# Second layer's routing logits in three column groups of TensorE, transposed once, with shorter rounds of work

## The chip, the cores and the metric

## The reference, cut to what matters

Banded attention (4 batches, 8 heads, 768 positions, 64 numbers a head) gives x, 3072 tokens of 512 numbers. Then a first layer of experts, each of which takes exactly 384 tokens in the order of all logits, and a second layer with free routing. The second layer's logits are what the change touches:

```python
def _moe2_ref(x, w_skip, w_gate, w1, w2):
    skip_score = x @ w_skip
    do_compute = skip_score > 0
    out = x.copy()
    xc = x[do_compute]
    logits = xc @ w_gate
    e_idx = np.argmax(logits, axis=1)
    ...
    for e in range(E):
        mask = e_idx == e
        h = np.maximum(xc[mask] @ w1[e], 0.0)
        y[mask] = gate_w[mask, None] * (h @ w2[e])
    out[do_compute] = xc + y
```

x there is the first layer's output. There are 8 experts (E), 512 features (DM, KC = 4 chunks of 128) and 1024 hidden numbers (F, FC = 8 chunks).

## The kernel before, in words

The program is one block with a hand-written stream of instructions for each engine; semaphores tie them. There is no scheduler: each engine does its instructions in the order in which they stand.

After the attention come eight **searches**, one for each expert of the first layer in the order in which they fill (`search` on VectorE, `window` on TensorE, from 166 to 573 us). A search finds the logit at which an expert has 384 tokens, in ROUNDS = 17 rounds. In a round VectorE counts how many logits reach each of three candidates (`junk`, L913), TensorE adds the counts over the partitions (L1370), and VectorE makes the next candidates. Then follow a total (L1380), the ranks of the chosen tokens (L1384, L1385), and the list of their ids (L1321, L1329). The next search starts with a transpose of the masked logits (L1364). `window` writes this down for TensorE, and between these steps it calls `work(units)`.

`work` takes items from the list WORK, in order, as long as their units fit into what `room` has allowed so far. WORK holds the first layer's products: 32 items "first" for an expert (L1297, 3 units each), 24 items "second" (L1311, 4 units), "rows" (L1286, the transposes of the gathered rows, 2 units each) and the items "tail", in which the second layer's logits are made. An expert has three tiles (CT = 3) of 128 tokens. The tail of expert k-1 stands among the first 16 items of expert k (`expert_items`): transposes of the output tiles `yb` into the PSUM tiles `XB`, copied by ScalarE to `yT` (`y_features`, L703), then the products of `yT` with the gate weights `wg2` into the PSUM tile `LP`, which ScalarE copies to L2 (L738). `wg2` has 9 real columns (8 experts and the skip weight), padded to 128 with zeros. The work lags behind the searches, so the tails of the first six experts are done in the searches three to eight, the seventh's after them, in `work(sum(...))`, and the eighth's at the end, between the halves of layer one of the second layer's first tile (L1421). Behind the seventh's tail stands the item "totals" (L1397), for which VectorE must have counted the tokens of the first 18 tiles; VectorE in turn waits (`tok_c`) for GpSimd's `keep_ids`, and that for the scatter of the seventh expert's outputs (L564).

The second layer takes tiles of 128 tokens, each with the weights of one expert: `layer1` (L1421, two halves), ScalarE's copies to `h2T` (L752), `x2_transpose` (L1410) and `layer2` (L1432).

Of the kernel before, what the change touches and what calls it, by code (L numbers as in the profile page):

```python
# [5 lines left out]
def banded_attention_two_moe_layers(nc, qT, kT, vwin, vblk, g1, w1a, w2a, skip2, g2, w1b, w2b, out):  # L6
    fp32, bf16, i32 = mybir.dt.float32, mybir.dt.bfloat16, mybir.dt.int32
    ALU = mybir.AluOpType
    ACT = mybir.ActivationFunctionType
# [6 lines left out]
    DM, E = g1.shape  # L16
# [19 lines left out]
    KC = DM // 128  # L36
    FC = F // 128
    CT = CAP // 128
# [6 lines left out]
    WIDE = 128  # L45
# [8 lines left out]
    ROUNDS = 17  # L54
# [5 lines left out]
    with ctx:  # L60
        def sb(name, shape, dt=fp32):
            return ctx.enter_context(nc.sbuf_tensor(name, shape, dt))
# [22 lines left out]
        wg1 = sb("wg1", [128, KC, WIDE + E * (TB - 1)])  # L85
        wg2 = sb("wg2", [128, KC, WIDE])

# [51 lines left out]
        def sba(name, shape, dt=fp32):  # L139
# [27 lines left out]
        yb = sb("yb", [128, CT, DM])  # L167
        yT = sb("yT", [128, 2, KC, 128])

# [58 lines left out]
            onehot_ready blk_ready id_mm idp_ready ids_ready tok_c  # L228
            xg_in xg_tr xgT_ready w_in0 w_in1 w2_in0 w2_in1 h_mm h_act y_mm y_evac y_tr yT_ready l2_mm l2_evac y_out y_st y_written
            gate_sub gate_exp rows8_ready base8_mm teA_ready onehot2_ready id2_mm gid2_ready route2_ready  # L230
# [408 lines left out]
        def _(act):  # L639
# [59 lines left out]
            def y_features(ph, j):  # L699
                act.wait_ge(s["y_tr"], CT * ph + j + 1)  # L700
                if j == 2:
                    act.wait_ge(s["l2_mm"], CT * ph + 1)
                a.activation(yT[:, j % 2, :, :], XB[(j + 1) % 2][:, :].rearrange("p (c t) -> p c t", c=KC),  # L703
                             ACT.Copy).then_inc(s["yT_ready"], 1)
# [10 lines left out]
            def expert(ph, last):  # L715
# [19 lines left out]
                if not last:  # L735
                    hidden(ph + 1, 1)
                act.wait_ge(s["l2_mm"], CT * (ph + 1))
                a.activation(L2[:, bass.ds(CT * ph, CT), :],  # L738
                             LP[:, 0:CT * (E + 1)].rearrange("p (j e) -> p j e", j=CT), ACT.Copy).then_inc(s["l2_evac"], 1)

# [423 lines left out]
        def _(pe):  # L1164
# [84 lines left out]
            def expert_items(k):  # L1249

                head = [("first", k, i, 3) for i in range(16)]
                if k > 0:
                    head[8:8] = [("tail", k - 1, 3, 4), ("tail", k - 1, 4, 4)]
                    head[4:4] = [("tail", k - 1, 1, 4), ("tail", k - 1, 2, 2)]
                    head[0:0] = [("tail", k - 1, 0, 4)]
# [15 lines left out]
            def room(w):  # L1271

                if w == 1:
                    return [0] + [0, 0, 6] + [6] * (ROUNDS - 3) + [15, 28, 4, 8]
                return [8] + [9] * ROUNDS + [15, 28, 4, 6 if w < 5 else 8]

# [158 lines left out]
            def tail(part, tp):  # L1435
# [13 lines left out]

                def y_logits(j):  # L1450
                    if j == 0:
                        pe.wait_ge(s["l2_evac"], START + tp)
                    pe.wait_ge(s["yT_ready"], START + CT * tp + j + 1)
                    for c in range(KC):
                        ins = mm(LP[:, (E + 1) * j:(E + 1) * j + WIDE], yT[:, j % 2, c, :], wg2[:, c, :],  # L1455
                                 start=(c == 0), stop=(c == KC - 1))
                    ins.then_inc(s["l2_mm"], 1)

                if part == 0:
                    y_transpose(0)  # L1460
                    y_transpose(1)
                elif part == 1:
                    y_logits(0)
                elif part == 2:
                    y_transpose(2)
                elif part == 3:
                    y_logits(1)
                elif part == 4:
                    y_logits(2)

# [6 lines left out]
            layer1(0, 0, 1, 0)  # L1477
            for part in range(1, 5):
                tail(part, E - 1)
            layer1(0, 0, 1, 1)  # L1480

            for b in range(KA):
# [60 lines left out]
```

## Time and profile before

| | us |
|---|---|
| median of 3 runs | 910.58 |
| lowest, highest | 905.64, 912.84 |
| the profiled execution, its time | 909.39 |
| its span, first to last instruction | 907.6 |
| TensorE busy in it | 860.7 |
| VectorE busy | 467.2 |
| ScalarE busy | 210.4 |
| GpSimd busy | 219.9 |

All profile times are from the one profiled execution, counted from the start of its span. "PE" is TensorE's matmuls, "PEld" its loads of stationary tiles. In a timeline a row is a run of like instructions: start, length until the last of them ends, engine, line, operation, tiles, stationary and moving shapes, count, and in brackets the idle time before it with what ended it. A window's row has, after its length, each engine's busy time with the number of its instructions, the granted clock of TensorE (1.00 is 2.4 GHz, 0.50 is 1.2 GHz), the DMA engines' share and GB/s.

### The profile page before, as it was taken

Reading aid. Unit: us, or ns where it says so; the run is one execution under the profiler, and the core shown is the slowest. Engines: PE = TensorE matmul, PEld = TensorE weight load, DVE = VectorE, ACT = ScalarE, POOL = GpSimd, SP = SyncE. Lnnn points to the kernel's source line nnn. Section 1 sums busy time; section 2 is a strip of 40 time slices with the busy share of each in tenths; the row PEclk is TensorE's granted clock in tenths of the full one; section 3 lists DMA queues with packets and bytes.
Section 4 is the critical chain, followed back from the end, with each engine's and each line's share of the span. In section 5 each row is a group of like instructions: output and inputs, shape, how many; then the busy total and the mean of one; then the engine's idle time right before and its main releaser. Section 6 shows DMA issues by size and latency. Waiting matters only on the chain.

```text
span 907.6 us, 15611 instructions
## 1 busy us (share of the span) xinstructions
PE 860.7 (95%) x5204; PEld 587.5 (65%) x5204; DVE 467.2 (51%) x2118; ACT 210.4 (23%) x662; POOL 219.9 (24%) x321
## 2 busy tenths in 40 slices
PE   4899999798899999999999999999999999999997
PEld 4789888686346455464646555564877776867775
DVE  8688886577777676667677676160270000000000
ACT  4456665320102121211202121221110111101010
POOL 3578875001030120203021020302012121212111
PEclk8799999899999999999999999999999999999999
DMA  7987751345070522507061431646788989888880
GB/s 206 273 234 213 228 162 48 116 164 188 33 257 34 198 92 89 189 12 266 24 239 51 163 126 56 220 178 208 238 291 324 344 311 337 304 333 321 316 299 15
DMA packets 69271, 174.78 MB, mean 193 GB/s; under 512 B 6064, under 2 KB 10672, under 8 KB 69216
## 3 DMA queue, kind: packets, MB, share of 16 engines
q1 hardware_dynamic: 54600, 143.99, 46.3%
q0 software_dynamic: 6960, 21.69, 6.9%
q10 hardware_dynamic: 7656, 8.36, 2.8%
q8 instruction: 35, 0.57, 0.3%
q14 instruction: 20, 0.16, 0.1%
HBM read 149.19 MB, written 23.59 MB: 190 GB/s over the span
## 4 chain that ended last, share of the span: by engine, by line
PE 78%; DVE 12%; DMA 5%; issue 3%; POOL 2%; ACT 1%; SPq 0%; DVEq 0%; POOLq 0%; ACTq 0%
PE bank L1297 15%; PE bank L1311 15%; PE bank L1421 14%; PE bank L1432 14%; DVE junk L913 3%; PE bank L1182 3%; PE bank L1204 3%; PE bank L1191 2%; PE bank L1455 2%; DMA vw<-vs 2%; PE bank L1218 2%; PE bank L1370 1%; DMA kc<-in_kT 1%; PE bank L1447 1%; PE bank L1286 1%
## 5 line engine op out<-in xcount | busy, mean ns | idle before, releaser
L1297 PE MATMUL bank<-xgT,W 128*128 128x384 f32 x512 | 179.9, 496 | 0.6 <-ACT xgT L686 0.6
L1311 PE MATMUL bank<-W,hT 128*128 128x512 f32 x384 | 178.8, 602 | 0.0
L913 DVE TENSOR_SCALAR_CACHE_REDUCE junk<-Vt,cand 128x192 bf16<-128x192 f32 x376 | 136.1, 410 | 4.8
L1421 PEld LDWEIGHTS bank<-x2T,W 128*128 128x128 f32 x1152 | 131.4, 192 | 7.7 <-issue 7.7
L1421 PE MATMUL bank<-x2T,W 128*128 128x128 f32 x1152 | 131.8, 275 | 0.0
L1432 PE MATMUL bank<-W,h2T 128*128 128x512 f32 x288 | 126.6, 592 | 0.0
L1297 PEld LDWEIGHTS bank<-xgT,W 128*128 128x128 f32 x512 | 90.3, 190 | 53.4 <-issue 3.6
L1070 DVE SCALAR_TENSOR_TENSOR o<-bank,gate,x 128x512 f32<-128x512 f32 x18 | 13.4, 750 | 211.6 <-PE bank L1432 211.6
L1311 PEld LDWEIGHTS bank<-W,hT 128*128 128x128 f32 x384 | 67.1, 190 | 58.0 <-issue 56.0
L1432 PEld LDWEIGHTS bank<-W,h2T 128*128 128x128 f32 x288 | 53.3, 190 | 60.3 <-issue 60.3
L651 ACT ACTIVATE pr<-bank,nmx 128x120 f32<-128x120 f32 x192 | 66.7, 364 | 34.2 <-DVE nmx L819 19.2
L752 ACT ACTIVATE h2T<-bank 128x512 f32<-128x512 f32 x36 | 21.5, 597 | 220.0 <-PE bank L1421 220.0
L691 ACT ACTIVATE hT<-bank 128x384 f32<-128x384 f32 x64 | 31.4, 490 | 150.3 <-PE bank L1297 150.3
L1182 PEld LDWEIGHTS bank<-kw,qz 128*128 128x128 f32 x384 | 55.8, 209 | 1.7
L471 POOL TENSOR_TENSOR pr<-pr,rinv 128x480 f32<-128x480 f32 x48 | 47.3, 985 | 33.4 <-DVE rinv L825 32.0
L1182 PE MATMUL bank<-kw,qz 128*128 128x120 f32 x384 | 55.2, 291 | 0.0
L280 POOL TENSOR_TENSOR hot_id<-hot,pnum 128x384 bf16<-128x384 f32 x7 | 8.2, 1166 | 186.7 <-DVE hot L977 186.7
L928 DVE TENSOR_SCALAR_CACHE_REDUCE reached<-bank 128x7 f32<-128x7 f32 x120 | 19.9, 166 | 62.1 <-PE bank L1370 60.2
L595 POOL COPY now_s<-sidx 128x1 int32 (+1 forms) x18 | 3.3, 183 | 193.3 <-DVE o L1070 193.3
L1370 PEld LDWEIGHTS bank<-cnt,same_e 128*128 128x128 bf16 x136 | 13.2, 97 | 50.7 <-DVE junk L913 45.1
L557 POOL DMA_INDIRECT xg<-x_rows,gidx x24 | 23.6, 985 | 91.3 <-DVE gidx L893 86.4
L564 POOL DMA_INDIRECT out<-yb,tok_i x24 | 23.6, 985 | 84.1 <-ACT yb L695 81.3
(262 smaller groups left out, 1076.8 us busy)
## 6 DMA issues: line engine op xcount, KB each, us to landing
W<-in_moe_w SPq DMA_DIRECT2D x52, 2048.0 KB, 8.0
vw<-in_vwin SPq DMA_DIRECT2D x16, 576.0 KB
qc<-in_qT SPq DMA_DIRECT2D x16, 384.0 KB, 6.6
kc<-in_kT SPq DMA_DIRECT2D x16, 384.0 KB, 7.8
vb<-in_vblk SPq DMA_DIRECT2D x16, 384.0 KB, 6.8
x_rows<-xr SPq DMA_DIRECT2D x24, 256.0 KB, 2.1
y_rows<-yb ACTq DMA_DIRECT2D x24, 256.0 KB
vw<-vs ACTq DMA_DIRECT2D x14, 144.0 KB
```

The lines of the kernel that those rows point to most:

```text
L471: g.tensor_tensor(pr[:, n % NP, :, :], pr[:, n % NP, :, :], rinv[:, n % NP, :].unsqueeze(2).to_broadcast([128, GW, KW]), ALU.mult) \
L557: g.indirect_dma_start(out=xg[:, j, :], out_offset=None, in_=x_rows, in_offset=bass.IndirectOffsetOnAxis(ap=gidx[:, j:j + 1], axis=0)) \
L564: g.indirect_dma_start(out=out, out_offset=bass.IndirectOffsetOnAxis(ap=tok_i[:, j:j + 1], axis=0), in_=yb[:, j, :], in_offset=None).then_ ...
L651: ins = a.activation(pr[:, n % NP, w, :], SC[n % 3][:, KW * w:KW * w + KW], ACT.Exp, scale=SCALE, bias=nmx[:, n % NP, w:w + 1], accum_out= ...
L691: a.activation(hT[:, r, :], HB[r % 2][:, 0:CAP], ACT.Relu).then_inc(s["h_act"], 1)
L913: ins = ve.tensor_scalar(junk[:, c, :], Vt[:, :], cand[:, c:c + 1].bitcast(fp32), 0.0, ALU.is_ge, ALU.add, accum_out=cnt[:, c:c + 1])
L1182: ins = mm(SC[n % 3][:, KW * w:KW * w + KW], qz[u % 2][:, GW * gr + w, :], kw[u % 2][:, GW * gr + w, :], start=False, stop=(w == GW - 1))
L1204: ins = mm(OB[n % 2][D * j:D * j + D, QW * w:QW * w + QW], vw[i][:, GW * gr + w, D * j:D * j + D], pT[:, n % 2, 128 * w + QW * j:128 * w + ...
L1297: ins = mm(HB[r % 2][:, 0:CAP], w1[:, c, 128 * r:128 * r + 128], xgT[:, c, :], start=(c == 0), stop=(c == KC - 1))
L1311: ins = mm(YB[j % 2][:, :], hT[:, r, 128 * j:128 * j + 128], w2[:, r, :], start=(r == 0), stop=(r == FC - 1))
L1421: ins = mm(HB2[h][:, 128 * c:128 * c + 128], W1[:, par, k * F + at:k * F + at + 128], x2T[par][:, k, :], start=(k == 0), stop=(k == KC - 1))
L1432: ins = mm(YB2[par][:, :], h2T[:, f, :], W2[:, par, f * DM:f * DM + DM], start=(f == 0), stop=(f == FC - 1))
```

## The change

The gate weights become the stationary operand, in 32 columns instead of 128, and `yT` the moving one. The three tiles of an expert write to partitions 0 to 31, 32 to 63 and 64 to 95 of `LP`, chunk by chunk in turn. ScalarE copies the 96x128 result to `l2T`, TensorE transposes it back, and ScalarE copies the real columns to L2. `yT` has three buffers instead of two. The tail has four parts instead of five: part 0 the transposes of two tiles, part 1 that of the third, part 2 all logits, part 3 the transpose of the result. They weigh 4, 2, 4 and 1 units instead of 4, 4, 2, 4 and 4, and stand before the first-layer items 0, 4, 8 and 10. The rounds' units alternate between 9 and 8 for fourteen rounds instead of always 9; the last entry of a search is 8 units but for the third search (4), where it was 6 for the third to fifth.

```diff
@@ -83,7 +83,8 @@
         iotaS = sb("iotaS", [128, NSLOT])
         cnt128 = sb("cnt128", [128, NT])
         wg1 = sb("wg1", [128, KC, WIDE + E * (TB - 1)])
-        wg2 = sb("wg2", [128, KC, WIDE])
+        wg2 = sb("wg2", [128, KC, 32])
+        l2T = sb("l2T", [CT * 32, 128])
 
 
         LM = sb("LM", [128, NT, E])
@@ -165,7 +166,7 @@
         xgT = sb("xgT", [128, KC, CAP])
         hT = sb("hT", [128, FC, CAP])
         yb = sb("yb", [128, CT, DM])
-        yT = sb("yT", [128, 2, KC, 128])
+        yT = sb("yT", [128, CT, KC, 128])
 
 
         R2 = sb("R2", [128, NT, NV, NSLOT], bf16)
@@ -226,7 +227,7 @@
             recip_ready norm_done sum_eps gaps_ready prob_tr prob_evac pv_done o_evac xr_tr xr_evac x_st0 x_st1 x_st2 x_st3
             logit_mm logit_in v_ready v_tr cnt_ready cnt_mm tau_diag tau_mm expert_ready expert_read rows_ready base_mm slot_ready
             onehot_ready blk_ready id_mm idp_ready ids_ready tok_c
-            xg_in xg_tr xgT_ready w_in0 w_in1 w2_in0 w2_in1 h_mm h_act y_mm y_evac y_tr yT_ready l2_mm l2_evac y_out y_st y_written
+            xg_in xg_tr xgT_ready w_in0 w_in1 w2_in0 w2_in1 h_mm h_act y_mm y_evac y_tr yT_ready l2_mm l2T_ready l2_tr l2_evac y_out y_st y_written
             gate_sub gate_exp rows8_ready base8_mm teA_ready onehot2_ready id2_mm gid2_ready route2_ready
             gidx_now sidx_now x2_in0 x2_in1 x2_in2 x2_in3 x2_tr x2T_ready te_ready h2_mm h2_act
             y2_mm o2_ready o2_out0 o2_out1 vec pool_c passed""".split()
@@ -698,9 +699,7 @@
 
             def y_features(ph, j):
                 act.wait_ge(s["y_tr"], CT * ph + j + 1)
-                if j == 2:
-                    act.wait_ge(s["l2_mm"], CT * ph + 1)
-                a.activation(yT[:, j % 2, :, :], XB[(j + 1) % 2][:, :].rearrange("p (c t) -> p c t", c=KC),
+                a.activation(yT[:, j, :, :], XB[(j + 1) % 2][:, :].rearrange("p (c t) -> p c t", c=KC),
                              ACT.Copy).then_inc(s["yT_ready"], 1)
 
             def gate_exp(first, count, n):
@@ -734,9 +733,12 @@
                 y_features(ph, 2)
                 if not last:
                     hidden(ph + 1, 1)
-                act.wait_ge(s["l2_mm"], CT * (ph + 1))
+                act.wait_ge(s["l2_mm"], ph + 1)
+                a.activation(l2T[:, :], LP[0:CT * 32, 0:128], ACT.Copy).then_inc(s["l2T_ready"], 1)
+                act.wait_ge(s["l2_tr"], ph + 1)
                 a.activation(L2[:, bass.ds(CT * ph, CT), :],
-                             LP[:, 0:CT * (E + 1)].rearrange("p (j e) -> p j e", j=CT), ACT.Copy).then_inc(s["l2_evac"], 1)
+                             LP[:, 128:128 + CT * 32].rearrange("p (j e) -> p j e", j=CT)[:, :, 0:E + 1],
+                             ACT.Copy).then_inc(s["l2_evac"], 1)
 
             x_features(0)
             hidden(0, 0)
@@ -1250,8 +1252,9 @@
 
                 head = [("first", k, i, 3) for i in range(16)]
                 if k > 0:
-                    head[8:8] = [("tail", k - 1, 3, 4), ("tail", k - 1, 4, 4)]
-                    head[4:4] = [("tail", k - 1, 1, 4), ("tail", k - 1, 2, 2)]
+                    head[10:10] = [("tail", k - 1, 3, 1)]
+                    head[8:8] = [("tail", k - 1, 2, 4)]
+                    head[4:4] = [("tail", k - 1, 1, 2)]
                     head[0:0] = [("tail", k - 1, 0, 4)]
                 items = head + [("first", k, i, 3) for i in range(16, HID)] + [("second", k, i, 4) for i in range(CT * FC)]
                 if k + 1 < E:
@@ -1272,7 +1275,7 @@
 
                 if w == 1:
                     return [0] + [0, 0, 6] + [6] * (ROUNDS - 3) + [15, 28, 4, 8]
-                return [8] + [9] * ROUNDS + [15, 28, 4, 6 if w < 5 else 8]
+                return [8] + [9, 8] * 7 + [9] * 3 + [15, 28, 4, 4 if w == 2 else 8]
 
             def load_x(k, j):
                 if j == 0:
@@ -1447,26 +1450,21 @@
                         ins = tr(XB[(j + 1) % 2][:, 128 * c:128 * c + 128], yb[:, j, 128 * c:128 * c + 128], ident[:, :])
                     ins.then_inc(s["y_tr"], 1)
 
-                def y_logits(j):
-                    if j == 0:
-                        pe.wait_ge(s["l2_evac"], START + tp)
-                    pe.wait_ge(s["yT_ready"], START + CT * tp + j + 1)
-                    for c in range(KC):
-                        ins = mm(LP[:, (E + 1) * j:(E + 1) * j + WIDE], yT[:, j % 2, c, :], wg2[:, c, :],
-                                 start=(c == 0), stop=(c == KC - 1))
-                    ins.then_inc(s["l2_mm"], 1)
-
                 if part == 0:
                     y_transpose(0)
                     y_transpose(1)
                 elif part == 1:
-                    y_logits(0)
+                    y_transpose(2)
                 elif part == 2:
-                    y_transpose(2)
+                    pe.wait_ge(s["l2_evac"], START + tp)
+                    pe.wait_ge(s["yT_ready"], START + CT * (tp + 1))
+                    for c in range(KC):
+                        for j in range(CT):
+                            ins = mm(LP[32 * j:32 * j + 32, 0:128], wg2[:, c, :], yT[:, j, c, :], start=(c == 0), stop=(c == KC - 1))
+                    ins.then_inc(s["l2_mm"], 1)
                 elif part == 3:
-                    y_logits(1)
-                elif part == 4:
-                    y_logits(2)
+                    pe.wait_ge(s["l2T_ready"], tp + 1)
+                    tr(LP[:, 128:128 + CT * 32], l2T[:, :], ident[0:CT * 32, 0:CT * 32]).then_inc(s["l2_tr"], 1)
 
             pe.wait_ge(s["const_ready"], 1)
             pe.wait_ge(s["const_in"], 32)
@@ -1475,9 +1473,10 @@
             work(sum(u for _, _, _, u in WORK))
             tail(0, E - 1)
             layer1(0, 0, 1, 0)
-            for part in range(1, 5):
-                tail(part, E - 1)
+            tail(1, E - 1)
+            tail(2, E - 1)
             layer1(0, 0, 1, 1)
+            tail(3, E - 1)
 
             for b in range(KA):
                 if b >= 1:
```

TensorE, rounds of the seventh search, before the change; `yb` is an output tile to be transposed, `wg,yT` the logits, `xgT,W` first-layer products:

```order
L1455 MATMUL bank<-wg,yT 128x128 x4
L1447 MATMUL bank<-ident,yb 128x128 x4
L1370 MATMUL bank<-cnt,same_e 128x128
L1297 MATMUL bank<-xgT,W 128x384 x3
L1370 MATMUL bank<-cnt,same_e 128x128
L1297 MATMUL bank<-xgT,W 128x384
L1455 MATMUL bank<-wg,yT 128x128 x8
L1370 MATMUL bank<-cnt,same_e 128x128
L1297 MATMUL bank<-xgT,W 128x384 x3
```

and with the change, where lines 1447, 1455, 1370, 1297 are 1450, 1463, 1373, 1300 and the logits' transpose is 1467:

```order
L1450 MATMUL bank<-ident,yb 128x128 x4
L1300 MATMUL bank<-xgT,W 128x384
L1373 MATMUL bank<-cnt,same_e 128x128
L1300 MATMUL bank<-xgT,W 128x384 x3
L1373 MATMUL bank<-cnt,same_e 128x128
L1463 MATMUL bank<-yT,wg 32x128 x12
L1300 MATMUL bank<-xgT,W 128x384
L1373 MATMUL bank<-cnt,same_e 128x128
L1300 MATMUL bank<-xgT,W 128x384
L1467 MATMUL bank<-ident,l2T 128x96
L1300 MATMUL bank<-xgT,W 128x384 x2
L1373 MATMUL bank<-cnt,same_e 128x128
```

The twelve calls of the logits are now in one round with one product, and the transpose is in the next.

TensorE, the seventh expert's tail and the first total (`row,tri`), before:

```order
L1447 MATMUL bank<-ident,yb 128x128 x8
L1297 MATMUL bank<-xgT,W 128x384 x4
L1455 MATMUL bank<-wg,yT 128x128 x4
L1447 MATMUL bank<-ident,yb 128x128 x4
L1297 MATMUL bank<-xgT,W 128x384 x4
L1455 MATMUL bank<-wg,yT 128x128 x8
L1397 MATMUL bank<-row,tri 128x8
L1398 MATMUL bank<-row,ones_bf 128x8
L1297 MATMUL bank<-xgT,W 128x384 x24
```

and with the change:

```order
L1450 MATMUL bank<-ident,yb 128x128 x8
L1300 MATMUL bank<-xgT,W 128x384 x4
L1450 MATMUL bank<-ident,yb 128x128 x4
L1300 MATMUL bank<-xgT,W 128x384 x4
L1463 MATMUL bank<-yT,wg 32x128 x12
L1400 MATMUL bank<-row,tri 128x8
L1401 MATMUL bank<-row,ones_bf 128x8
L1300 MATMUL bank<-xgT,W 128x384 x2
L1467 MATMUL bank<-ident,l2T 128x96
L1300 MATMUL bank<-xgT,W 128x384 x22
```

The first total now has all logits before it and their transpose, with two products, behind it.

TensorE, the eighth expert's tail among the second layer's first tile (`x2T,W`), before:

```order
L1447 MATMUL bank<-ident,yb 128x128 x8
L1421 MATMUL bank<-x2T,W 128x128 x16
L1455 MATMUL bank<-wg,yT 128x128 x4
L1447 MATMUL bank<-ident,yb 128x128 x4
L1455 MATMUL bank<-wg,yT 128x128 x8
L1421 MATMUL bank<-x2T,W 128x128 x16
L1410 MATMUL bank<-ident,x_1 128x128 x4
L1432 MATMUL bank<-W,h2T 128x512 x8
```

and with the change:

```order
L1450 MATMUL bank<-ident,yb 128x128 x8
L1424 MATMUL bank<-x2T,W 128x128 x16
L1450 MATMUL bank<-ident,yb 128x128 x4
L1463 MATMUL bank<-yT,wg 32x128 x12
L1424 MATMUL bank<-x2T,W 128x128 x16
L1467 MATMUL bank<-ident,l2T 128x96
L1413 MATMUL bank<-ident,x_1 128x128 x4
L1435 MATMUL bank<-W,h2T 128x512 x8
```

The logits now follow the third tile's transposes at once, and their own transpose stands behind the second half of layer one.

ScalarE at the same place, before:

```order
L697 DMA y_rows<-yb 128x512
L703 ACTIVATE yT<-bank 128x512 x3
L738 ACTIVATE L<-bank 128x27
L752 ACTIVATE h2T<-bank 128x512 x2
L712 ACTIVATE x2T<-bank 128x512
L708 ACTIVATE t<-t 128x48
```

and with the change:

```order
L698 DMA y_rows<-yb 128x512
L702 ACTIVATE yT<-bank 128x512 x3
L737 ACTIVATE l2T<-bank 96x128
L739 ACTIVATE L<-bank 128x27
L754 ACTIVATE h2T<-bank 128x512 x2
L711 ACTIVATE x2T<-bank 128x512
L707 ACTIVATE t<-t 128x48
```

The copy to `l2T` is added; it and the copy to L stand ahead of the first copy to `h2T`.

## Rows read from the trace of the kernel before

**Rows 1.** The page: the chain that ended last, by engine.
```profile
PE 78%; DVE 12%; DMA 5%; issue 3%; POOL 2%; ACT 1%; SPq 0%; DVEq 0%; POOLq 0%; ACTq 0%
```

**Rows 2.** TensorE in windows: the third, the fourth and the seventh search.
```profile
263.45:315.52 52.07, 51.11 (x216) 1.00 0.35 126
315.52:367.18 51.66, 50.70 (x215) 1.00 0.36 125
470.33:521.91 51.58, 51.20 (x216) 1.00 0.36 130
```

**Rows 3.** TensorE's timeline, rounds of the seventh search.
```profile
478.61 0.22 PE L1370 MATMUL bank<-cnt,same_e 128*128 128x128 bf16 x1
...
480.42 0.23 PE L1370 MATMUL bank<-cnt,same_e 128*128 128x128 bf16 x1 [0.29 <-DVE junk L913]
...
493.01 0.22 PE L1370 MATMUL bank<-cnt,same_e 128*128 128x128 bf16 x1
...
493.77 1.95 PE L1455 MATMUL bank<-wg,yT 128*128 128x128 f32 x16
495.55 0.22 PE L1370 MATMUL bank<-cnt,same_e 128*128 128x128 bf16 x1
...
497.60 0.22 PE L1370 MATMUL bank<-cnt,same_e 128*128 128x128 bf16 x1
```

**Rows 4.** TensorE's timeline, a group of the attention.
```profile
80.69 0.69 PE L1204 MATMUL bank<-pT,vw 120*64 120x64 f32 x16 [0.25 <-DMA vw<-vs]
```

**Rows 5.** TensorE's timeline, around the rank matmuls of that search.
```profile
512.69 5.31 PE L1311 MATMUL bank<-W,hT 128*128 128x512 f32 x12
517.93 0.77 PE L1321 MATMUL bank<-hot_blk,hot_id 128*32 128x24 bf16 x24
518.62 1.13 PE L1311 MATMUL bank<-W,hT 128*128 128x512 f32 x2
```

**Rows 6.** The chain of waits: start, length, what.
```profile
589.18 4.51 DMA out<-yb,tok_i
...
614.13 5.15 PE bank L1311 x12
```

**Rows 7.** TensorE's timeline, the seventh expert's last routing logits.
```profile
594.94 1.95 PE L1455 MATMUL bank<-wg,yT 128*128 128x128 f32 x16
598.34 0.18 PE L1397 MATMUL bank<-row,tri 128*128 128x8 bf16 x1 [1.45 <-DVE row L1081]
```

**Rows 8.** TensorE's timeline, the last expert's routing logits.
```profile
640.88 0.60 PE L1447 MATMUL bank<-ident,yb 128*128 128x128 f32 x4
641.32 2.01 PE L1455 MATMUL bank<-wg,yT 128*128 128x128 f32 x16
...
647.17 7.03 PE L1432 MATMUL bank<-W,h2T 128*128 128x512 f32 x16
```

**Rows 9.** ScalarE's timeline, the same place.
```profile
641.52 0.60 ACT L703 ACTIVATE yT<-bank 128x512 f32<-128x512 f32 x1 [3.68 <-PE bank L1447]
...
643.45 0.59 ACT L752 ACTIVATE h2T<-bank 128x512 f32<-128x512 f32 x1
```

**Rows 10.** TensorE's timeline, four of its waits.
```profile
15.58 0.36 PE L1179 MATMUL bank<-band,spread 67*128 67x480 bf16 x1 [2.17 <-DVE kw L800]
...
34.08 1.12 PE L1204 MATMUL bank<-pT,vw 120*64 120x64 f32 x16 [2.35 <-issue]
...
166.14 0.30 PE L1364 MATMUL bank<-ident,V 128*128 128x128 f32 x1 [3.03 <-DVE V L900]
...
216.94 0.23 PE L1370 MATMUL bank<-cnt,same_e 128*128 128x128 bf16 x1 [1.48 <-DVE junk L913]
```

**Rows 11.** Windows: all engines; PEclk is TensorE's granted clock.
```profile
16.60:26.70 10.10, 7.17 (x43) 6.24 (x42) 7.63 (x20) 4.71 (x25) 6.28 (x8) 0.50 0.55 161
33.70:40.40 6.70, 6.32 (x50) 5.78 (x51) 4.49 (x11) 3.01 (x15) 5.67 (x8) 0.50 1.04 276
166.80:173.50 6.70, 5.48 (x27) 5.42 (x28) 3.98 (x25) 2.14 (x4) 0.00 (x0) 0.50 0.21 78
```

## The prediction

> **What bounds the kernel now.** I read the chain that ended last first: TensorE holds 78% of it, VectorE 12% [rows 1]. So a TensorE microsecond is worth one wherever TensorE is not waiting, and the question is where it would wait. The windows tell that. From the third search on, a search with an expert's products woven in takes 51.6 to 52.1 us, of which TensorE is busy 50.7 to 51.2, at full granted clock [rows 2]. The timeline of the seventh search shows what sets a round. A round begins with the count matmul (L1370); VectorE then tests three candidates, while TensorE works off the round's units. Where TensorE has little to do it waits for VectorE's `junk`: the round from 478.61 to 480.42 is 1.81 us, with 0.29 us of visible wait. That is the floor of a round. A round of three first-layer products takes 2.05 us (495.55 to 497.60); the round with one such product and eight logit calls (16 records) takes 2.54 (493.01 to 495.55) [rows 3]. Hence a first-layer product costs about 0.65 us and the count matmul about 0.11. A second-layer product is 0.86 (12 records in 5.15) [rows 6].
>
> There are eight places with routing logits, one for each expert. Six of them (experts one to six) lie in the rounds of searches three to eight; the seventh and the eighth come after the searches, and they behave differently.
>
> **What the change removes and adds, for one expert.** Removed: 12 calls that load a 128x128 stationary tile and move 128 columns, 24 records. 16 of them take 1.78 us from 493.77 to 495.55 [rows 3], so 0.111 each and 2.67 for 24. Added: 12 calls with 32 stationary columns and 128 moving ones, writing to three partition groups, then a transpose of one record.
>
> The trace has no call with 32 stationary float columns. The nearest is the attention's product with the values, 64 stationary and 64 moving columns, in two partition groups in turn. Its 16 records are busy for 0.69 us, the last of them for about 0.22, so they start within 0.47, 0.03 apart [rows 4]. In a single row 64 columns would take half of 0.111, 0.056. So two streams do run side by side, with float data. They read about as much in a unit of time as three streams with 32 weight columns would: there 256 numbers of a partition (2 x 64 weights, 2 x 64 moving) in 0.06 us, here 480 (3 x 32 and 3 x 128) in 0.111. I take three streams side by side: 8 steps of 0.111 make 0.89. Bounds: nothing side by side, 24 x 0.111 = 2.67; all records at the attention's spacing, 24 x 0.03 = 0.72.
>
> Going over to narrow stationary tiles has a price. The rank matmuls (L1321, 32 columns wide) start 5.24 us after 12 second-layer records that elsewhere take 5.15 [rows 5, 6], so 0.09 to go over; I take 0.09 again for the way back. The logits then cost 1.07 (0.90 to 2.85). The added transpose is one record, 0.11 (four take 0.44) [rows 8]. **Saved: 2.67 - 1.18 = 1.49 us an expert.** Eight times that, 11.9, is the most the change can give.
>
> At TensorEngine Tiling (Array Packing), section Key Properties, the Trainium skill says that a change of tiling mode drains TensorE; the 0.09 in [rows 5, 6] agrees. The Trainium skill's page TensorE: Matmul & The Clock Gate, section Measured speedup vs the span model, gives 2.38 times for three column tiles, not 3. By that the eight steps would be 1.12 instead of 0.89, and the sum below some 1.6 us less gain.
>
> **In the rounds of searches three to eight.** By the order of instructions a whole search holds the same set of products before and after, so TensorE's work falls by 1.49, but its waits at the floor grow. Before, the seventh search has one short round (four row transposes and one second-layer product: 0.44 + 0.86 + 0.11 = 1.41 against 1.81, 0.40 of waiting). After, it has that one and a second, with only two first-layer products: 0.11 + 1.30 = 1.41, another 0.40. The round with the new logits and one product is 0.11 + 1.07 + 0.65 = 1.83, just on the floor: a faster stream gives nothing there, a slower one costs one for one. Net 1.49 - 0.40 = 1.1 for each of searches five to eight, 4.3 together. The cuts of searches three and four fall on other items. The third saves 1.49 and gives a second-layer product (0.86) to the fourth, but two of its rounds fall partly under the floor and its end comes before VectorE's next masked logits: an estimated 0.6 to 0.7 of waiting, net 1.7. The fourth saves 1.49, takes that product, and loses the wait of about 0.4 with which it ends now: 1.1. **Sum 7.1 us.** The sections after the rounds stay as they are from the fifth search on.
>
> What hides the new steps: ScalarE must copy 96x128 numbers between logits and transpose. Two first-layer products and a count matmul stand between, 1.4 us; the copy starts some 0.25 after the last matmul and takes under 0.6, as ScalarE's copy of 512 columns does [rows 9]. I cost it at nothing; uncovered it would be 0.8 for each expert. The three `yT` buffers remove one wait of ScalarE and add none. SyncE's and GpSimd's queues get nothing new. VectorE's smaller fill of `wg2` at the start lies before a wait for the first keys: nothing.
>
> **The seventh expert.** Here TensorE waits already: after the last logits 1.45 us, until 598.34, for VectorE's `row` [rows 7]. The chain behind goes over the scatter of expert seven's last output tile (a DMA of 4.51 us) [rows 6], then `tok_i` on GpSimd and VectorE's counting. None of it is shortened. TensorE arrives 1.6 us earlier (1.49, and the transpose now stands two products behind the wait) and waits 1.6 longer: 3.05 us. Gain zero, and the transpose behind it is a loss of 0.11.
>
> **The eighth expert.** Now one set of logits follows its transposes at once, all three tiles needed: `yT` is ready 0.64 after the transposes start plus 0.60 [rows 8, 9], so TensorE stands about 0.7. It had stood 0 there. Logits 1.07, 32 records, the transpose. Then a new tie: ScalarE is in order, and its copy of the first half of `h2T`, now at 643.45 [rows 9], stands behind the copy of the logits, that is behind the transpose after the second half of layer one. The half ends near 641.3 + 1.07 + 3.57 (32 records of 0.111) = 645.9; with the transpose, the copies and their delays ScalarE frees `h2T` at about 646.9, and the second-layer products start near 646.95 instead of 647.17 [rows 8]. Gain 0.2 of a possible 1.49. VectorE gets the last logits some 2.9 us later, at 646.4. The second total wants its counting only behind the first tile's second-layer products, which last 7.03 us from 647.17 [rows 8]; the same counting, GpSimd's copies with it, took 4.7 us from the end of the DMA (593.7) to 598.34 [rows 6, 7]. It fits.
>
> Sum: 7.1 - 0.1 + 0.2 = **7.2 us off**, if the clock holds.
>
> **The granted clock.** The wait grown to 3.05 us is a matter of its own. The windows show TensorE at 0.50, its lower level of 1.2 GHz instead of 2.4, in three stretches [rows 11], and each begins just after a long wait: of 2.17, 2.35 and 3.03 us [rows 10]. After waits of 1.48 [rows 10] and 1.45 [rows 7] the clock stays whole. So the widened wait probably sends the clock down. The shortest such stretch is 6.8 us (166.8 to 173.5) [rows 11]; after this wait TensorE has nothing but products ahead, so half of it is lost, 3.4, less what falls into the wait itself: 3.3. Net: 7.2 - 3.3 = 3.9 us off.
>
> **Rivals.**
> - The clock falls (likeliest, 50%): own time 909.39, 907.6 of it span, becomes 905.5. The median of the runs is 1.2 above the profiled run, so 906.7. For it: three waits of over 2 us, three falls. Against: only three.
> - The clock holds (20%): 903.4.
> - The three streams don't run side by side, so the change doesn't do what it says (10%). Logits 2.85 instead of 1.07, 1.78 dearer. Six times in the rounds 10.7; no gain and no fall at the seventh expert, whose wait is then 1.3; 1.7 at the eighth: 12.4 - 7.2 = 5.2 slower, **915.8**. It decides from about 2.1 us for one set of logits. Against it: [rows 4].
> - ScalarE's copy isn't hidden or the streams are a quarter dearer than 0.89, and the clock falls (10%): 1.5 to 5 us less gain, 908 to 911.
> - More gain than seen, since the scatter ends earlier or the rounds' waits are shorter (10%): 900 to 902.
>
> **How the numbers follow.** The forecast is the likeliest case, 906.7. The range takes in both clock cases, the dearer streams and part of the extra gain, and a spread like that of the three runs (905.64 to 912.84) around the middle: 901 to 911.5. It leaves out the case without overlap. A measurement of this kernel can tell about 1% from no change, 9.1 us. Over 1% faster needs more than my whole sum: 0.14. Within: 0.81. Slower by over 1% needs no overlap and more: 0.05.
>
> **What the profile after would show.** Right: 24 records of the logits in 0.9 to 1.0 us, in threes; a search of 50.5 us; a wait near 3 us before the first total (now L1400); a window at PEclk 0.50 after it; about 0.7 of waiting before the eighth logits. Wrong: single spacing of 0.11 for the logits, a wait before the transpose `l2T`, searches that shrink by less than 0.8, or a whole clock after 600.

## The result and the profile after

The changed kernel takes 902.36 us in the median of nine runs (897.85 to 909.16), the kernel before, run beside it nine times, 912.84 (905.64 to 915.83). The ratio is 0.9893 with a 95% interval of 0.9859 to 0.9927: 9.8 us less, between 6.7 and 12.9. That is inside the range on record and 4.3 us below the forecast, near the case in which the clock holds (903.4). The likeliest case on record, a fall of the clock, did not come in the profiled execution.

The profiled execution took 897.85, the fastest of the nine; its span is 896.1 against 907.6. Not all of these 11.5 us are the change's. The attention and the first two searches, which it leaves as they are, end at 260.11 instead of 263.45; in twelve more executions of relatives of both kernels that point lay between 260.0 and 265.1. So the profiles are compared from the first matmul of the third search to the end: 644.1 us before, 636.0 after, **8.1 less**.

TensorE in windows, changed kernel, the third, the fourth and the seventh search, cut at each search's first matmul as in [rows 2]:

```profile
260.11:310.58 50.47, 49.08 (x215) 1.00 0.36 130
310.58:361.22 50.64, 50.07 (x216) 1.00 0.36 130
462.40:512.99 50.59, 50.02 (x217) 1.00 0.36 134
```

52.07, 51.66 and 51.58 have become 50.47, 50.64 and 50.59. TensorE's timeline in the seventh search, changed kernel, which answers to [rows 3]; L1373 is the count matmul, L1463 the logits, L1467 their transpose:

```profile
472.50 0.23 PE L1373 MATMUL bank<-cnt,same_e 128*128 128x128 bf16 x1 [0.24 <-DVE junk L915]
...
484.85 0.22 PE L1373 MATMUL bank<-cnt,same_e 128*128 128x128 bf16 x1
485.00 1.07 PE L1463 MATMUL bank<-yT,wg 128*32 128x128 f32 x24
486.00 0.91 PE L1300 MATMUL bank<-xgT,W 128*128 128x384 f32 x2
486.75 0.22 PE L1373 MATMUL bank<-cnt,same_e 128*128 128x128 bf16 x1
...
487.51 0.25 PE L1467 MATMUL bank<-ident,l2T 96*128 96x96 f32 x1
...
492.76 0.23 PE L1373 MATMUL bank<-cnt,same_e 128*128 128x128 bf16 x1 [0.24 <-DVE junk L915]
```

The 24 records of the logits are busy for 1.07 us; the next product starts 1.00 after their start, where 24 took 2.67 before. The round with them is 1.90 us (484.85 to 486.75). Two rounds end in a wait of 0.24 us for VectorE's `junk`, at 472.50 and 492.76; before, one did.

The chain of waits over the seventh expert's last output tile, changed kernel, which answers to [rows 6], and TensorE's timeline there, which answers to [rows 7]:

```profile
579.26 2.72 DMA out<-yb,tok_i
...
586.63 0.18 PE bank L1400
```

```profile
584.22 1.07 PE L1463 MATMUL bank<-yT,wg 128*32 128x128 f32 x24
586.63 0.18 PE L1400 MATMUL bank<-row,tri 128*128 128x8 bf16 x1 [1.33 <-DVE row L1083]
```

The wait before the first total is 1.33 us, not 3.05, because the scatter took 2.72 us instead of 4.51. TensorE's clock stayed whole. The queues while the scatter was under way, first the kernel before (589.2 to 593.5), then the changed one (579.3 to 582.2); columns are packets, MB and the share of the 16 DMA engines:

```profile
q0 software_dynamic: 80, 0.26, 16.4%
q10 hardware_dynamic: 144, 0.26, 16.2%
q8 instruction: 1, 0.02, 2.2%
```

```profile
q10 hardware_dynamic: 144, 0.26, 24.1%
q0 software_dynamic: 80, 0.26, 23.7%
```

The data packets are the same, 80 of the scatter and 144 of the copy to `y_rows`. In the kernel before one packet of the instruction queue (16 KB) fell among them.

TensorE's timeline at the eighth expert's tail, changed kernel, which answers to [rows 8]:

```profile
628.39 0.60 PE L1450 MATMUL bank<-ident,yb 128*128 128x128 f32 x4
629.77 1.07 PE L1463 MATMUL bank<-yT,wg 128*32 128x128 f32 x24 [0.78 <-ACT yT L702]
...
635.56 4.96 PE L1435 MATMUL bank<-W,h2T 128*128 128x512 f32 x11 [0.42 <-ACT h2T L754]
```

Two waits stand there that were not there before: 0.78 us for `yT` and 0.42 for `h2T`.

### The profile page after: what moved, and what is told of

Its sections match the earlier page's. It is cut to its first block, busy times and chain, and to the rows that moved or that the text cites. A ratio compares the mean times of both kernels' runs of the same rounds, so it can differ in the third digit from the quotient of the medians.

```text
span 896.1 us, 15627 instructions
## 1 busy us (share of the span) xinstructions
PE 849.3 (95%) x5212; PEld 569.7 (64%) x5212; DVE 466.4 (52%) x2118; ACT 212.1 (24%) x670; POOL 220.2 (25%) x321
## 4 chain that ended last, share of the span: by engine, by line
PE 79%; DVE 13%; DMA 3%; issue 3%; POOL 2%; ACT 1%; DVEq 0%; POOLq 0%; SPq 0%; ACTq 0%
PE bank L1314 15%; PE bank L1300 15%; PE bank L1424 14%; PE bank L1435 14%; DVE junk L915 4%; PE bank L1184 4%; PE bank L1206 3%; PE bank L1193 3%; PE bank L1220 2%; PE bank L1373 2%; DMA vw<-vs 1%; PE bank L1289 1%; PE bank L1450 1%; PE bank L1413 1%; PE bank L1181 1%
## 5 line engine op out<-in xcount | busy, mean ns | idle before, releaser
L1300 PE MATMUL bank<-xgT,W 128*128 128x384 f32 x512 | 182.3, 497 | 0.6 <-ACT xgT L687 0.6
L1314 PEld LDWEIGHTS bank<-W,hT 128*128 128x128 f32 x384 | 66.8, 190 | 58.4 <-issue 56.5
L1184 PEld LDWEIGHTS bank<-kw,qz 128*128 128x128 f32 x384 | 55.9, 209 | 1.7
L1373 PEld LDWEIGHTS bank<-cnt,same_e 128*128 128x128 bf16 x136 | 13.2, 97 | 57.8 <-DVE junk L915 54.3
```

Source lines behind the costliest of these rows:

```text
L1184: ins = mm(SC[n % 3][:, KW * w:KW * w + KW], qz[u % 2][:, GW * gr + w, :], kw[u % 2][:, GW * gr + w, :], start=False, stop=(w == GW - 1))
L1300: ins = mm(HB[r % 2][:, 0:CAP], w1[:, c, 128 * r:128 * r + 128], xgT[:, c, :], start=(c == 0), stop=(c == KC - 1))
L1314: ins = mm(YB[j % 2][:, :], hT[:, r, 128 * j:128 * j + 128], w2[:, r, :], start=(r == 0), stop=(r == FC - 1))
L1373: mm(CNT, same_e[:, :], cnt[:, :].unsqueeze(1).to_broadcast([128, WIDE // 8, 8]), start=True, stop=True).then_inc(s["cnt_mm"], 1)
```

## The experiments

Each edit is to the changed kernel unless it says otherwise. "From the third search" means from its first matmul to the end of the span; the changed kernel has 636.0 there, the kernel before 644.1 and, in the second execution below, 644.1.

**e1_serial: one partition group after the other.**

```diff
-                    for c in range(KC):
-                        for j in range(CT):
+                    for j in range(CT):
+                        for c in range(KC):
                             ins = mm(LP[32 * j:32 * j + 32, 0:128], wg2[:, c, :], yT[:, j, c, :], ...)
```

> The changed kernel with the two loops of the logits swapped: all four chunks of one tile, then the next tile, so the next call mostly goes to the same partition group. Theory (three streams run side by side because the groups alternate): the 24 records now take about 24 x 0.111 = 2.7 us, busy 2.8 instead of 1.07; a round with the logits and one product grows from 1.90 to about 3.5, a search from 50.59 to about 52.2; six searches and the eighth expert cost 1.6 to 1.7 each, the seventh 0.3 to 1.7: 10 to 13 us slower than the changed kernel, at or above the kernel before. Rival (the order of the calls doesn't matter, the 32-column loads are what is cheap): 24 records in 1.0 to 1.2 us, no difference in time.

The ratio to the kernel before is 0.9993 (0.9963 to 1.0022). Same place in the seventh search, TensorE's timeline:

```profile
491.28 2.00 PE L1463 MATMUL bank<-yT,wg 128*32 128x128 f32 x24
493.21 0.91 PE L1300 MATMUL bank<-xgT,W 128*128 128x384 f32 x2
```

The 24 records now take 1.93 us to the next product, not 1.00 and not 2.7. The round is 2.82 us instead of 1.90, a search 51.5 instead of 50.6, and from the third search it is 643.8, 7.8 more than the changed kernel. Not all of it is the order's: the wait before the first total is 1.84 us here, since the seventh expert's last scatter is slow again, 4.16 us, and that makes 1.4 of the 7.8 (e9 and e12 show why). The other 6.4 are the order of the calls alone: 5.5 in the six searches, 0.9 at the eighth expert. So the rival falls. The kernel before has the slow scatter too, and against it this order gains only 0.3 us from the third search on. But the theory's size was too large. Eight records of one group at 0.11 are 0.87, three such streams end to end 2.6; they took 1.93, so each stream began some 0.35 us before the one ahead of it had ended, although its calls stand behind. The starts of the single records agree: by their spacing, the second group's first record starts at 491.75 and the first group's last at 492.07.

**e2_wait3, e10_wait3again, e11_wait4: a longer wait before the first total.**

```diff
-            WORK.insert(WORK.index(("first", E - 1, 8, 3)), ("totals", 0, 0, 1))
+            WORK.insert(WORK.index(("first", E - 1, 7, 3)), ("totals", 0, 0, 1))
```

e11_wait4 has 6 in place of 7; e10_wait3again is e2_wait3 once more.

> The changed kernel with the item totals one product and the logits earlier, before the seventh of the first products of the last expert. Its wait for VectorE must grow from 1.33 us to 1.33 + 0.65 + 1.07 = 3.05 us. Theory of the prediction (a wait of about 3 us sends the granted clock down): a stretch at 0.50 of 3.4 us or more begins within some 3 us of the wait; 1.7 us are lost to the wait and 1.7 to 3.4 to the clock, 3.4 to 5.1 slower than the changed kernel in the runs where it falls. Rival (waits amid dense products are harmless, those at the start were something else): wait of 3.05, PEclk 1.00 after it, 1.7 us slower. If the scatter of expert seven takes 4.4 to 4.7 us instead of 2.9, as in the profiled execution of the kernel before, the wait is 4.8.

> The same kernel as e2_wait3, to see another wait of 3.0 us before the first total. If the length of a wait alone decides, the granted clock stays at 1.00 as it did there. If it hangs on where the wait falls, it may drop to 0.50 this time, for 3.4 to 6.8 us, and the time to the second total grows from 57.7 us by 1.7 to 3.4.

> The totals one product earlier still: the wait becomes 3.6 us. Theory (waits from about 3.5 us on always send the clock down, those near 3 sometimes): PEclk 0.50 behind it for 3.4 us or more, and 58.4 + 1.7 to 3.4 us from the first total to the second. Rival (the clock falls only after waits at which the products before were already thin): PEclk 1.00, 58.4 us.

e2_wait3 took 904.75 in the median of five, ratio 0.9929 (0.9889 to 0.9970). Its wait, and TensorE in a window behind it (the column after the engines is the granted clock):

```profile
586.54 0.18 PE L1400 MATMUL bank<-row,tri 128*128 128x8 bf16 x1 [2.98 <-DVE row L1083]
```

```profile
586.60:596.00 9.40, 9.40 (x52) 5.62 (x53) 7.87 (x38) 2.24 (x6) 0.00 (x0) 1.00 0.56 198
```

e10_wait3again, the same program:

```profile
590.07 0.19 PE L1400 MATMUL bank<-row,tri 128*128 128x8 bf16 x1 [2.99 <-DVE row L1083]
```

```profile
589.30:596.10 6.80, 6.03 (x32) 3.30 (x33) 5.74 (x25) 0.76 (x2) 0.00 (x0) 0.50 0.21 58
```

and e11_wait4, behind a wait of 3.64 us:

```profile
589.60:592.80 3.20, 3.20 (x16) 1.45 (x18) 2.79 (x14) 0.49 (x1) 0.00 (x0) 0.50 0.00 0
```

One wait of 2.98 left the clock whole, one of 2.99 was followed by 6.8 us at half, one of 3.64 by 3.4 us. From the first total to the second it is 57.7, 60.6 and 60.0 us; without a fall 57.7 and an expected 58.4. So a fall cost 2.8 us where it lasted 6.8 (the prediction had 3.3) and 1.6 where it lasted 3.4. The price was about as forecast, but a wait near 3 us doesn't decide by its length. In these three executions the scatter took 2.7 us.

**e3_open: nothing between the logits and their transpose.**

```diff
-                    head[10:10] = [("tail", k - 1, 3, 1)]
-                    head[8:8] = [("tail", k - 1, 2, 4)]
+                    head[8:8] = [("tail", k - 1, 2, 4), ("tail", k - 1, 3, 1)]
```

> The changed kernel with the transpose of the logits directly behind them, so that nothing covers ScalarE's copy to l2T. Theory (the two products and the count matmul hide the copy): the profile shows 0.4 to 0.6 us of TensorE waiting for ScalarE before the transpose, seven times; a search grows by 0.3 to 0.6, the sum is 2 to 4 us, about 0.3 per cent, and only the profile can tell. Rival (the round's floor hides it anyway, since VectorE is still counting): the wait is seen, but the round stays below 2.0 us and a search at 50.6.

```profile
491.51 0.30 PE L1466 MATMUL bank<-ident,l2T 96*128 96x96 f32 x1 [0.38 <-ACT l2T L737]
```

TensorE waits 0.38 us for ScalarE in a search (0.22 in the third), and a search takes 51.0 instead of 50.6; from the third search it is 638.0, 2.0 more. Two products are enough cover: in the changed kernel the wait is not there.

**e4_oldunits: the rounds' units of the kernel before.**

```diff
-                return [8] + [9, 8] * 7 + [9] * 3 + [15, 28, 4, 4 if w == 2 else 8]
+                return [8] + [9] * ROUNDS + [15, 28, 4, 6 if w < 5 else 8]
```

> The changed kernel with the rounds' units of the kernel before: 9 in each round, 6 or 8 at the end. Theory (the tail weighs 7 units less, so with the old allowance the products run ahead of the searches by 5 to 7 units each, until the rows of the next expert are asked for before the gather has brought them): waits of TensorE for the DMA of xg appear from the fifth search on, 1 to 7 us each, in all 8 to 15 us slower than the changed kernel. Rival (the units only shift work between rounds): no waits for xg, time within 2 us of the changed kernel.

935.32 us, ratio 1.0234 (1.0185 to 1.0284). TensorE's list of waits, and its timeline at the one of the eighth search:

```profile
PE bank L1289 <- DMA xg<-x_rows,gidx: 26.1, 7, 6.9
```

```profile
547.65 1.12 PE L1289 MATMUL bank<-ident,xg 128*128 128x128 f32 x4 [6.44 <-DMA xg<-x_rows,gidx]
```

The mechanism is the one expected, the size is not: 26.1 us of waits for the gathered rows. They grow from 0.63 us in the fourth search over 2.94, 3.88 and 4.86 to 6.44 in the eighth and 6.86 behind it, and from the fifth search on 3.4 to 6.8 us at half clock follow each. Searches five to seven take 57.8, 56.8 and 59.0 us, and from the third search to the end it is 670.4, 34.4 more than the changed kernel, where 8 to 15 were expected. The units are not decoration: without the smaller allowance the cheaper tail makes the kernel slower than it was before the change, by 2.3%, some 21 us (17 to 26).

**e5_late: the first total four products later.**

```diff
-            WORK.insert(WORK.index(("first", E - 1, 8, 3)), ("totals", 0, 0, 1))
+            WORK.insert(WORK.index(("first", E - 1, 12, 3)), ("totals", 0, 0, 1))
```

> The changed kernel with the item totals four first-layer products later, before the twelfth of the last expert. Theory (the 1.33 us before the first total are VectorE's chain over the scatter, and there is room behind it): no wait before the first total or only that of a slow scatter, the list matmuls still don't wait, 1.3 us less from the last search to the end. Rival (the lists then come late): TensorE waits for VectorE's one-hots before the list matmuls, as long as was won.

```profile
589.14 1.48 PE L1300 MATMUL bank<-xgT,W 128*128 128x384 f32 x4
590.46 0.17 PE L1400 MATMUL bank<-row,tri 128*128 128x8 bf16 x1
```

No wait is left, neither there nor before the lists. From the eighth search's first matmul to the second total it is 128.2 us, 129.5 in the changed kernel: 1.3 less.

**e6_halves: the eighth tail spread over the halves of layer one.** `layer1` takes the range of its column blocks as a new argument; its own lines are left out here.

```diff
-            layer1(0, 0, 1, 0)
+            layer1(0, 0, 1, 0, range(0, 2))
             tail(1, E - 1)
+            layer1(0, 0, 1, 0, range(2, 4))
             tail(2, E - 1)
-            layer1(0, 0, 1, 1)
+            layer1(0, 0, 1, 1, range(0, 2))
             tail(3, E - 1)
+            layer1(0, 0, 1, 1, range(2, 4))
```

> The changed kernel with the eighth expert's tail spread over the halves of layer one: eight calls stand between the third tile's transposes and the logits, and eight after the logits' transpose. Theory (0.78 us of waiting for yT and 0.42 us for h2T are ties of this order alone): both waits gone, 1.2 us less from the seventh expert to the end. Rival (ScalarE is the limit there, so the wait moves): one of them stays at 0.3 us or more.

Both waits are gone. From the first total to the second it takes 54.4 us instead of 55.9: 1.5 less, a little more than the two waits.

**e7_units: rounds without short ones.** A search's 18 numbers of units for the rounds are written out, with the same sum:

```diff
-                return [8] + [9, 8] * 7 + [9] * 3 + [15, 28, 4, 4 if w == 2 else 8]
+                if w == 2:
+                    return [6, 9, 8, 9, 6, 9, 9, 9, 8, 8, 8, 9, 9, 12, 9, 10, 8, 8] + [15, 28, 4, 4]
+                return [8, 8, 8, 7, 10, 8, 12, 6, 9, 9, 8, 8, 11, 8, 8, 11, 4, 11] + [15, 28, 4, 8]
```

> The changed kernel with other units for the rounds of searches three to eight, same sums: no round below VectorE's floor of 1.81 us but the one before the last count, whose floor is 1.41 since only one candidate is tested. Theory (in the changed kernel each search loses 0.4 us in each of two short rounds and up to 0.1 in others): a search falls from 50.59 to about 49.8, six of them 4.5 us, about 0.5 per cent faster than the changed kernel. Rival (VectorE's chain as a whole bounds a search, and the time turns up in the sections after the rounds): the rounds shrink but the search stays within 0.2 us of 50.6.

TensorE in the seventh search:

```profile
464.55:514.32 49.77, 49.68 (x218) 1.00 0.37 132
```

49.77 us, 0.82 less, and TensorE busy but for 0.1. The six searches gave 4.5 us together, as expected, and from the third search it takes 631.5. The time, 899.65 in the median of four, ratio to the kernel before 0.9881 (0.9851 to 0.9911), doesn't separate it from the changed kernel's 0.9893.

**e8_all: the edits of e5_late, e6_halves and e7_units together.**

> The three edits together: the units without short rounds, the totals four products later, the eighth tail spread over the halves. If each does what its own experiment should show, 4.5 + 1.3 + 1.2 = 7 us less than the changed kernel: a ratio to the kernel before near 0.981. Rival (they meet in the same slack): 0.985 or more.

898.14 us in the median of six, ratio 0.9854 (0.9828 to 0.9880). From the third search 628.7 us: 7.3 less than the changed kernel, 15.5 less than the kernel before. In the profile the three gains add up as the theory has it; the ratio of the times is not the 0.981 expected but stands where the rival put it, at 0.985 or more, and why the times show less than the profile stays open. Its interval still overlaps that of the changed kernel (0.9859 to 0.9927), so the times alone don't separate the two; the stretch from the third search on, 644.1 in both executions of the kernel before, does, and it is the shortest of all here.

**e9_before: the kernel before once more.**

> The kernel before once more, for a second profiled execution. Theory (the 4.8 us of expert seven's last scatter and the wait of 1.45 us behind it were particular to the first execution; the scatter mostly takes 3.0): scatter 3.0, no wait or under 0.2 us before the first total, 75.0 us from the eighth search's first matmul to the first total instead of 76.4. The part from the third search's first matmul to the end is then 642.7 us against 636.0 in the changed kernel, 6.7 apart. Rival (that wait belongs to the kernel before): scatter 4.5 or more and the wait of 1.45 again. The first matmul of the third search lies between 260 and 265 as in the changed kernel's profiles; if it comes at 267 or later, the change has shortened the attention.

The theory falls. Span 907.0, from the third search 644.1 again; the third search began at 262.9, so the attention wasn't shortened. TensorE waited 1.39 us before the first total, and the scatter behind it, in the chain of waits, was slow again:

```profile
588.61 4.44 DMA out<-yb,tok_i
```

```profile
q8 instruction: 1, 0.02, 2.1%
```

The packet of the instruction queue is there again. e1_serial has it too, with a scatter of 4.2 us to landing; all eleven executions without such a packet on this scatter have 2.7.

**e12_shift: the kernel before, the instruction packet moved.**

```diff
                     if w == 1 and n < 2:
                         keep_busy(0, 6)
+                    if w == 1 and 5 <= n < 15:
+                        mm(LP[:, 0:128], ident[:, :], ident[:, :], start=True, stop=True)
```

> The kernel before with ten more float matmuls on TensorE (identity by identity into the idle tile LP, 40 instructions) in the second search, one in each of ten rounds that leave TensorE 0.33 us of waiting. The result is not used. Theory (the seventh expert's last scatter is slow, 4.4 to 4.8 us instead of 3.0, because a 16 KB packet of the instruction queue falls on it, and that packet comes when TensorE's program has come to a certain place): 40 instructions more bring the packet 3 to 5 us forward, before the scatter; the scatter takes 3.0, the wait before the first total goes from 1.4 to under 0.2, and the time from the eighth search's first matmul to the first total from 76.4 to about 75.0. Rival (the slow scatter comes from something else that the tail's order sets, as the traffic of the y rows): packet moved, scatter still 4.4 or more and 76.4 us.

The packet now falls between 578 and 582, the scatter starts at 587.33. The queues from 587.3 to 590.4:

```profile
q10 hardware_dynamic: 144, 0.26, 22.3%
q0 software_dynamic: 80, 0.26, 22.1%
...
out<-yb,tok_i POOLq DMA_INDIRECT x1, 2.7
```

and TensorE at the first total:

```profile
593.09 1.95 PE L1457 MATMUL bank<-wg,yT 128*128 128x128 f32 x16
594.87 0.17 PE L1399 MATMUL bank<-row,tri 128*128 128x8 bf16 x1
```

2.7 us to landing, no wait, and 74.8 us from the eighth search's first matmul to the first total instead of 76.4. The ten matmuls were added to the second search alone, and behind the eighth 1.6 us came back. It is the packet that makes the scatter slow. What sets the packet's time is less sure. The one before it came 290.6 and 290.4 us after the third search's first matmul in the two executions of the kernel before and 283.8 here, so more instructions on TensorE did bring that one forward. The one at the scatter came after 327.3 and 327.2 us, and here after 317.4; but e2_wait3 and e10_wait3again are one program, their searches are alike to 0.02 us, and it came after 327.6 in one and 317.7 in the other. A shift of 10 us happens without any edit.

## Why the prediction was right, and where not

**The bound and the price of the logits: right.** TensorE was the bound, and the rounds came out as read, to 0.1 us. The logits cost 1.00 to the next product and 0.09 to go over to narrow tiles (the count matmul stands 0.15 before them and 0.06 before others), 1.09 against 1.07 on record; the transpose 0.08 against 0.11. Three streams do run side by side (e1_serial). By the Trainium skill's factor of 2.38 (TensorE: Matmul & The Clock Gate, section Measured speedup vs the span model) the logits would cost an estimated 1.3 instead of the 1.09. Here three groups in turn made 24 records, 2.67 us before, 1.00, and the measurement decides.

**The six searches: right, 6.6 for 7.1.** By search 1.60, 1.02, 0.97, 1.00, 1.00 and 1.00, where 1.7, 1.1 and four times 1.1 stood. The second short round took its 0.4 as said. The term was large by 0.1 each since the round with the logits is 1.90 and not 1.83.

**The seventh expert: wrong.** The step was "None of it is shortened": TensorE would arrive 1.6 us earlier and wait 1.6 longer. It did arrive earlier, but the chain ended 1.8 us earlier too. Its largest piece, the scatter's 4.51 us, was no fixed latency: 2.7 us of it are the scatter's own, the rest came from an instruction packet that crossed it (e9, e12). Whether the change moved the packet off or it fell elsewhere by chance stays open: both executions of the kernel before have it there, and of the changed kernel and its ten variants only e1_serial, but in one program it moves by 10 us (e2, e10). So 1.8 us of the 8.1 have nothing to do with cheaper logits; e12 gets 1.6 of them in the kernel before with ten matmuls whose results nobody reads. With no packet on the scatter in either kernel, 642.5 in e12 against 636.0, the change is worth 6.5 us, where 7.2 stood for a clock that holds.

**The clock: a sound mechanism without its cause.** The forecast rested on a wait of 3.05 us, and the wait was 1.33. The 3.3 us that stood for a fall were not spent, and with the 1.8 above they are why the time came out below the forecast; it is in the range because the range took in both clock cases. e10 and e11 show that such a wait can send the clock down and what it costs; e2 shows that it need not. Of the three waits of 2.94 to 2.99 us among the experts' products (e4, e2, e10) two came with a fall, and so did the wait of 3.03 us before the first search in all fourteen executions. The five in seven that the rivals gave a fall is not contradicted, and not shown either.

**The eighth expert: the sign of a small term.** Forecast 0.2 gained. From the first total to the second the changed kernel takes 55.9 us against 55.7, 0.17 more, of which the seventh expert's transpose is 0.08: 0.1 lost. The waits were seen (0.7 and the tie of `h2T`; 0.78 and 0.42 measured), their sum was 0.3 too small.

Together: 6.6 + 1.8 - 0.2 = 8.2 by these pieces, 8.1 from the third search to the end, and 9.8 (6.7 to 12.9) by the times. What of the last 1.7 is more than scatter of the measurement stays open; no part of either kernel before the third search differs beyond what repeats of one kernel differ.

## What to carry to other kernels

Where narrow outputs leave most of TensorE's columns idle, let calls to different partition groups follow each other in turn: in turn 24 records took 1.00 us, group after group 1.93. When a woven stream gets cheaper, give the plan of work new numbers at once and look at each round against the other engine's floor: kept numbers cost 34 us from the third search on here, and better ones gave 4.5. Before you take a DMA's latency from one execution as fixed, compare it with its siblings: 4.5 us where most like it took 2.7 was a collision with a packet that can fall 10 us earlier in the next execution.

## What the runs showed of the hardware

Packets of the instruction queue share the DMA engines with data. One of 16 KB on a scatter of 80 packets stretched it from 2.7 to between 4.2 and 4.5 us in all three executions in which one fell on expert seven's last tile. With ten matmuls added to TensorE's program 350 us earlier it fell elsewhere, once, which is within the 10 us by which it moves in one program. How much a packet costs hangs on where in the scatter it falls: in those three it came 1.4 to 1.5 us after the scatter's start. In the changed kernel one came 1.9 us into a scatter that starts at 369.31, which took 4.3, and one 2.5 us into that at 429.04, which took 3.0; in e12_shift one came 0.2 us before that at 579.18, which took 3.1.

Calls to another partition group start before the ones ahead of them are done: in e1_serial three streams of eight records, written one behind the other, overlapped by about 0.35 us each.

The granted clock fell at waits of 2.94 us (e4_oldunits) and 2.99 (e10_wait3again), and not at one of 2.98 in the same program as the latter (e2_wait3). Each fall among the experts' products lasted 3.4 or 6.8 us.
